# Scores of chunks 5 to 11 of an mLSTM and gated-FFN kernel: fp32 matmuls replaced by stacked fp32r ones

## What is computed

```python
for t in range(S):                      # mLSTM, per batch and head; 2 x 8 heads, S = 768, D = 40
    m_new = np.maximum(f + m, i)
    f_stab, i_stab = np.exp(f + m - m_new), np.exp(i - m_new)
    C = f_stab * C + i_stab * outer(vt, kt);  n = f_stab * n + i_stab * kt
    y[t] = sigmoid(o) * (C @ qt) / max(abs(n @ qt), 1)
x = y as 1536 tokens x 320
x = (1 / (1 + np.exp(-(x @ w_gate))) * (x @ w_val)) @ w_out      # 320 -> 1536 -> 320
return ((x @ w_a) * (x @ w_b)) @ w_out2                          # the same, without a sigmoid
```

## Time and profile before

| | us |
|---|---|
| median of 3 runs (485.88 to 488.06) | 486.16 |
| the profiled execution | 485.53 |
| its span in the trace | 483.7 |
| PE busy | 470.9 (97%) |
| ACT busy | 182.9 (38%) |
| DVE busy | 175.7 (36%) |
| POOL busy | 110.7 (23%) |

### The profile page before, as it was taken

How to read it: one execution, slowest core, us unless ns; L and a number is a source line. 1 busy time by engine, 2 the same in 40 slices (tenths; PEclk the granted TensorE clock), 3 DMA queues, 4 the chain that set the end, 5 groups by cost and what they waited for, 6 DMA issues and landing times.

```text
span 483.7 us, 6541 instructions
## 1 busy us (share of the span) xinstructions
PE 470.9 (97%) x2531; PEld 412.4 (85%) x2531; DVE 175.7 (36%) x339; ACT 182.9 (38%) x345; POOL 110.7 (23%) x97
## 2 busy tenths in 40 slices
PE   7968899999999999999999999999999999999997
PEld 4867789888898988988888888888888888888886
DVE  6754534343454433334322234222222222222223
ACT  4544574643527263423434444222232222222222
POOL 3348855561230302000344443000000000000000
PEclk9996999999999999999999999999999999999999
DMA  5675837423141326000123310000010000100001
GB/s 136 210 216 158 241 125 247 124 68 102 47 132 55 99 74 210 1 0 1 47 93 108 123 47 1 0 1 0 1 55 1 0 1 0 56 1 1 0 1 54
DMA packets 20890, 34.34 MB, mean 71 GB/s; under 512 B 2372, under 2 KB 15068, under 8 KB 20860
## 3 DMA queue, kind: packets, MB, share of 16 engines
q1 hardware_dynamic: 20231, 32.93, 21.8%
q10 hardware_dynamic: 629, 1.00, 0.6%
HBM read 31.85 MB, written 2.04 MB: 70 GB/s over the span
## 4 chain that ended last, share of the span: by engine, by line
PE 89%; DMA 5%; POOL 2%; SPq 2%; issue 1%; DVE 0%; POOLq 0%; DVEq 0%
PE bank L518 53%; PE bank L535 26%; PE bank L446 3%; PE bank L421 3%; DMA levels<-a_scratch 1%; DMA vk<-vk_in 1%; DMA i_row<-i_in 1%; PE bank L437 1%; DMA d_scratch<-d_row 1%; PE bank L500 1%; PE bank L486 1%; DMA bmask<-bm_in 1%; PE bank L459 1%; PE bank L470 1%; POOL w_lo L1008 1%
## 5 line engine op out<-in xcount | busy, mean ns | idle before, releaser
L848 DVE TENSOR_TENSOR h_ff<-bank,s_ff 128x512 f32<-128x512 f32 x72 | 49.8, 691 | 194.3 <-PE bank L518 185.8
L518 PE MATMUL bank<-xt,w_hi 128*128 128x512 f32 x360 | 118.5, 394 | 1.4 <-issue 1.4
L679 ACT CAST h_hi<-h_ff 128x512 fp32r<-128x512 f32 x72 | 44.6, 619 | 133.0 <-DVE h_ff L848 129.9
L672 ACT ACTIVATE s_ff<-bank 128x512 f32<-128x512 f32 x72 | 43.1, 599 | 133.5 <-PE bank L518 133.3
L518 PE MATMUL bank<-xt,w_lo 128*128 128x512 f32 x216 | 84.7, 392 | 0.0
L518 PEld LDWEIGHTS bank<-xt,w_hi 128*128 128x128 f32 x360 | 65.6, 188 | 13.3 <-issue 1.8
L854 DVE TENSOR_TENSOR h_lo<-h_ff,h_hi 128x512 fp32r<-128x512 f32 x72 | 52.1, 724 | 55.4 <-ACT h_hi L679 55.4
L518 PE MATMUL bank<-xt,w_hi_mid 128*128 128x512 f32 x180 | 59.2, 394 | 0.0
L518 PE MATMUL bank<-xt,w_hi_end 128*128 128x512 f32 x180 | 59.2, 394 | 0.0
L518 PEld LDWEIGHTS bank<-xt,w_lo 128*128 128x128 f32 x216 | 40.5, 188 | 8.7
L535 PE MATMUL bank<-w_hi,h_hi 128*128 128x320 f32 x144 | 45.2, 314 | 0.0
(11 more groups left out here) (106 smaller groups left out, 660.7 us busy)
## 6 DMA issues: line engine op xcount, KB each, us to landing
w_raw<-w_in SPq DMA_DIRECT2D x24, 544.0 KB, 4.2
vk<-vk_in SPq DMA_DIRECT2D x12, 344.0 KB, 3.2
levels<-a_scratch SPq DMA_DIRECT2D x8, 512.0 KB
k<-kq_in SPq DMA_DIRECT2D x11, 180.0 KB
y<-rows_t SPq DMA_DIRECT2D x12, 160.0 KB, 1.9
q<-kq_in SPq DMA_DIRECT2D x10, 180.0 KB
q_blk<-q_in SPq DMA_DIRECT2D x22, 60.0 KB
osig_b<-o_in SPq DMA_DIRECT2D x8, 160.0 KB, 3.2
```

The costliest lines, as they stand in the source:

```text
L518: mm = pe.matmul(up_bank(u, gv)[:, :], w_part(low, f, (gv * 3 + kt) * P, P), xt[:, xb * TOK + g * TG:xb * TOK + (g + 1) * TG], start=(j == ...
L672: act.activation(s_ff[u % 2][:, :], up_bank(u, 0)[:, :], ACT.Sigmoid if u < UNITS // 2 else ACT.Copy).then_inc(act_s, 1)
L679: act.copy(h_hi[u % 2][:, :], h_ff[u % 2][:, :]).then_inc(act_h, 1)
L848: dve.tensor_tensor(h_ff[u % 2][:, :], up_bank(u, 1)[:, :], s_ff[u % 2][:, :], ALU.mult).then_inc(dve_h, 1)
```

## The change

Chunks 5 to 11 get another form of the scores. Queries and keys of a chunk are loaded in plain form into `part_raw`, ACT rounds them to fp32r (`part_high`), POOL takes the rest (`part_low`), and SP stores both parts to DRAM (`store_part`). From there SP reads them back stacked along the contraction (`load_stack`): per head 120 partitions hold for the keys high, high, low, and for the queries high, low, high. One fp32r matmul per head, contraction 120, 128 columns, then gives high x high + high x low + low x high. Per chunk this is two loads, two stores and six stacked loads in place of four loads.

`q_stk` and `k_stk` lie where the `q_blk` and `k3` of chunk 4 lay. `part_high` stands on ACT at k = 1 (queries) and k = 2 (keys), behind `h_high`; `part_low` on POOL in the same units, ahead of `w_low`. To make room, `osig_b`, `s_ff` and `h_ff` have one buffer instead of two, with waits to match (the last four lines of the diff are those of `gate(u)` and `hidden(u)`), and `rec` shares `den`.

```diff
+            def load_part(n, q_or_k):
+                rows, width = part_of(q_or_k)
+                wait(sp, pool_part, part_no(n, q_or_k) - 1)
...
+                sp.dma_start(part_raw[0:rows, 0:width], src).then_inc(ld_part, 16)
+            def store_part(n, q_or_k):
+                rows, width = part_of(q_or_k)
+                sp.wait_ge(pool_part, part_no(n, q_or_k))
...
+                sp.dma_start(dst, src.bitcast(F32)).then_inc(st_part, 16)
+            def load_stack(n, q_or_k):
+                sp.wait_ge(pe_s, 2 * n)
+                sp.wait_ge(st_part, 16 * part_no(n, q_or_k))
+                for at in range(3):
...
+                    sp.dma_start(dst.bitcast(F32), src).then_inc(ld_stk, 16)
...
             load_w(4)
-            load_o(5)
+            load_part(ALONE + 1, "q")
             for u in range(3 * (NCH - ALONE) - 2):
                 n, k = piece(u)
-                if k == 0 and n >= ALONE + 2:
+                if k == 0:
                     load_o(n)
+                    store_part(n, "k")
+                    load_stack(n, "k")
+                    if n + 1 < NCH:
+                        load_part(n + 1, "q")
                 if k == 1 and n + 1 < NCH:
                     load_rows(n + 1)
-                    load_q(n + 1)
+                    store_part(n + 1, "q")
+                    load_part(n + 1, "k")
                 if k == 2 and n + 1 < NCH:
                     load_scaled(n + 1)
                     load_v(n + 1)
+                    load_stack(n + 1, "q")
...
+                if n > ALONE:
+                    for h in range(half * HEADS // 2, (half + 1) * HEADS // 2):
+                        at, k_at = (h - half * HEADS // 2) * P, (h % 3 * 3 + h // 3) * P
+                        mm = pe.matmul(st[:, at:at + P], k_stk[:, k_at:k_at + P], q_stk[:, h * P:(h + 1) * P],
+                                       start=True, stop=True)
...
+            def part_high(n, q_or_k):
+                rows, width = part_of(q_or_k)
+                act.wait_ge(ld_part, 16 * part_no(n, q_or_k))
+                wait(act, st_part, 16 * (part_no(n, q_or_k) - 1))
+                act.copy(part[0:rows, 0:width], part_raw[0:rows, 0:width]).then_inc(act_part, 1)
...
+            def part_low(n, q_or_k):
+                pool.wait_ge(act_part, part_no(n, q_or_k))
+                pool.tensor_tensor(part[0:rows, width:2 * width], part_raw[0:rows, 0:width],
+                                   part[0:rows, 0:width].bitcast(F32), ALU.subtract).then_inc(pool_part, 1)
...
-                wait(act, dve_h, u - 1)
+                wait(act, dve_h, u)
-                wait(dve, act_h, u - 1)
+                wait(dve, dve_hlo, u)
```

More of the change, by code:

```diff
@@ L102, in ab @@
                 return stack.enter_context(nc.sbuf_tensor(f"{name}{s}", shape, dt))
+            if s == 0:
+                stacks = ExitStack()
+                stacked.append(stacks.enter_context(nc.sbuf_tensor("q_stk", [TRI, HEADS * P], F32R)))
+                stacked.append(stacks.enter_context(nc.sbuf_tensor("k_stk", [TRI, TRI // HD * 3 * P], F32R)))
+                stacks.close()
+            q_tile, k_tile = ab("q_blk", [TRI, HEADS * P]), ab("k3_", [TRI, 3 * P])
+            if s == 0:
+                ab("k_rest", [TRI, 6 * P])
             rows = ExitStack()
@@ L135, in build @@
         set0 = chunk_set(ctx, 0)
-        levels, arow, q_blk, k3, q3, i_rep, vk, pt, x_raw, x_n, den, rec = zip(set0, set1)
+        levels, arow, q_blk, k3, q3, i_rep, vk, pt, x_raw, x_n, den = zip(set0, set1)
+        q_stk, k_stk = stacked
+        part_raw, part = sb("part_raw", [P, 3 * P]), sb("part", [P, 6 * P], F32R)
         w_hi, w_lo = sb("w_hi", [P, 6 * WC], F32R), sb("w_lo", [P, 6 * WC], F32R)
@@ L139, in build @@
         w_raw = [sb(f"w_raw{i}", [P, WC]) for i in range(RING)]
-        consts = sb("consts", [P, 2 * P])
-        ident = consts[:, 0:P]
-        osig_b = [sb(f"osig_b{i}", [P, DM]) for i in range(2)]
+        ident = sb("ident", [P, P])
+        osig_b = sb("osig_b", [P, DM])
         d_row, m_prev = sb("d_row", [ROWS, CHUNKS]), sb("m_prev", [ROWS, CHUNKS])
@@ L152, in build @@
         h_lo = [sb(f"h_lo{i}", [P, TG], F32R) for i in range(2)]
-        s_ff = [sb(f"s_ff{i}", [P, TG]) for i in range(2)]
-        h_ff = [sb(f"h_ff{i}", [P, TG]) for i in range(2)]
+        s_ff, h_ff = sb("s_ff", [P, TG]), sb("h_ff", [P, TG])
         bank = [ctx.enter_context(nc.psum_tensor(f"bank{i}", [P, 512], F32)) for i in range(8)]
@@ L678, in h_high @@
                 wait(act, pe_d, u - 1)
[L679 removed]
+                act.copy(h_hi[u % 2][:, :], h_ff[:, :]).then_inc(act_h, 1)
             def rows_out(group):
@@ L699, in _ @@
             act.wait_ge(dve_warm, 1)
-            act.activation(s_ff[0][0:1, 0:1], h_hi[0][0:1, 0:1].bitcast(F32), ACT.Sigmoid).then_inc(act_table, 1)
+            act.activation(s_ff[0:1, 0:1], h_hi[0][0:1, 0:1].bitcast(F32), ACT.Sigmoid).then_inc(act_table, 1)
             act.wait_ge(dve_zero, 2)
@@ L747, in _ @@
                 h_high(u)
+                if k in (1, 2) and n + 1 < NCH:
+                    part_high(n + 1, " qk"[k])
                 if k == 0:
@@ L816, in combine @@
                 dve.wait_ge(dve_den, 2 * n + 2)
-                dve.reciprocal(rec[s][:, :], den[s][:, :]).then_inc(dve_rec, 1)
+                dve.reciprocal(den[s][:, :], den[s][:, :]).then_inc(dve_rec, 1)
                 dve.wait_ge(dve_rec, n + 1)
@@ L820, in combine @@
                 dve.tensor_tensor(heads(x_raw[s][:, :], HD), u3[:, :, 0:HD],
-                                  rec[s][:, :].unsqueeze(2).to_broadcast([P, HEADS, HD]),
+                                  den[s][:, :].unsqueeze(2).to_broadcast([P, HEADS, HD]),
                                   ALU.mult).then_inc(dve_y, 1)
@@ L974, in open_x @@
                 s = set_of(n)
-                gate, at = (osig_a, n * DM) if n < ALONE else (osig_b[n % 2], 0)
+                gate, at = (osig_a, n * DM) if n < ALONE else (osig_b, 0)
                 pool.wait_ge(act_o, 1 if n < ALONE else n - 2)
@@ L1066, in _ @@
                         mask(n + 1)
+                if k in (1, 2) and n + 1 < NCH:
+                    part_low(n + 1, " qk"[k])
                 for f in W_AT.get(u, ()):
```

50 lines of the change are left out of this document (38 added, 12 removed).

## The result

The changed kernel took 522.38 us (median of 4 runs, 518.36 to 523.3) against 486.8 for the kernel before: a ratio of 1.0718, 95% interval 1.0673 to 1.0762. The forecast was 487.0, its range 481.5 to 493.5. It was wrong in size and in kind: no rival reached beyond 497. The profiled execution took 523.3 us, its span is 521.5. Executions that ran over 1.5% longer than the fastest of their kernel (one each in runs 4, 5 and 8) are left out of all ratios.

What follows compares the result with a forecast made beforehand. PE almost alone was taken to bound the kernel from 58 us on. A saving of 6.0 us against waits of 1.1, 1.2, 2.5, 1.4 and 1.1 gave +1.3 us, forecast as 487.0 us, range 481.5 to 493.5.

Steps and rivals of the forecast that it cites:

- The saving: Scores of chunks 5 to 11: fp32r matmuls at 0.109 us, 0.87 a chunk instead of 1.73, 6.0 us saved.
- rival 1: Scores' matmuls faster, 0.064 us each: 8.5 us saved, 484.5 us in all; chance 0.15.
- rival 2: Scores' narrow fp32r matmuls run at the fp32 rate: nothing saved, only the waits, 493 us; chance 0.15.
- (a): PE waits for open_x(4), delayed on POOL behind chunk 5's query split: 1.1 us (bounds 0.4 and 1.6).
- (b): Weight load w(6) issued late behind the queries' store, so gate(2) holds up PE: 1.2 us (bounds 0 and 2.5).
- (c): Chunk 5's scores wait for the keys' stack, loaded behind w(6): 2.5 us (bounds 0 and 4).
- (d): Chunk 6's scores wait for the keys' stack: 1.4 us (bounds 0 and 3.4).
- (e): Chunks 7 to 11: round trip of 9.0 against 8.6 to 8.9 us given, waits of 1.1 (bounds 0 and 12).
- stacks 4.0: Time for a chunk's three key stack loads, 552 KB, within the round trip before its scores: 4.0 us.
- rival 3: Keys' store takes 5.0 us rather than 3.0, so five chunks wait 2 more each: 497 us; chance 0.08.
- The rest: Other edits, such as single buffers for s_ff, h_ff and osig_b and rec in den, were to cost nothing.
- the bound of 10: Sign across the kernel: the forecast is wrong if the waits sum to less than 5 or more than 10 us.

Runs made afterwards that it cites:

- run 4: Changed kernel with the new form in chunks 6 to 11 only, splits one unit earlier, stack loads at k = 2, weight loads ahead of stores: 487.39 us.
- run 5: Run 4 with the new form from chunk 7 on, loads of weights 12 on held, tiles aligned: 482.31 us; with chunk 6 also in the new form: 484.24.
- run 8: Kernel before with key and query loads of chunks 5 to 11 issued late: 505.3 us, again 511.26; with loads released later still: 533.58.
- run 1: Changed kernel's buffers, tile places and waits, with the loads and fp32 scores of the kernel before: 488.18 us, ratio 1.0046.
- run 6: d_row allocated ahead of w_hi, which moves tile starts by 32 bytes: 488.04 us in the kernel before, 520.65 in the changed kernel.
- run 2: Changed kernel with parts made for chunk 5 only; chunks 6 to 11 load chunk 5's stacks early: 491.48 us, ratio 1.0121.
- Run 3: Changed kernel with 7 to 17 extra matmuls of 512 columns ahead of each stack wait: 514.26 us, ratio 1.0581.
- run 7: Changed kernel with loads of stale keys, in differently split groups, measured by themselves after chunk 11's scores: 525.04 us, once.

## Why the prediction was wrong, step by step

- **What bounds the kernel: right.** PE alone; every late datum was lost whole.
- **The saving: right.** 0.106 us a matmul, 0.88 a chunk; rivals 1 and 2 fall with it.
- **(a) open_x(4), 1.1:** PE waited 3.2 for it, 1.8 above before. But the wait scatters: kernels with before's order there waited 1.4 to 2.7 (2.1 in the mean of eight traces: before, runs 1, 4, 5, 6 and 8), those with the changed order 2.5 to 3.2 (3.0 in five: after, runs 2, 3, 6 and 7). So some 0.8 is the change's, and the step was about right.
- **(b) w(6), 1.2:** right in mechanism, and 1.5 measured. Its cast began at 70.39 with ACT idle 6.58 before it, not near 67, but PE came as much later. A second weight block was late in the same way (PE waited 2.0 for its gate until 101.48), which no term had.
- **(c) and (d), keys of chunks 5 and 6, 2.5 and 1.4:** measured 4.0 and 4.2. The store landed in 7.7 and 6.0 us, priced as bytes in a backlog at some 2.0 each, and the stack load took 6.4 and 6.6 where I had 4.0 (for 552 KB; three loads of 180 are 540, which changes 0.1 us).
- **(e) chunks 7 to 11, 1.1 in sum:** measured 3.5 + 1.8 + 1.6 + 1.5 + 1.8 = 10.2. The term that failed is "stacks 4.0". The stacks took 6.4, 5.2, 5.3, 5.2 and 5.6, together 7.7 over, most of the 9.1 that the term was short. The store was right (2.9 in four of five; 3.5 in chunk 7). The 4.0 came from a line through two landings, a store's of 160 KB and a load's of 344 KB; alone a load of 180 KB takes 2.7 to 3.1 here. A round trip of 9.0 against a lead of 8.6 to 8.9 is decided by its error; I should have put far more on rival 3. That rival had the size of the waits (10) but the wrong leg and a chance of 0.08.
- **The step that is missing: what a wait costs beyond itself.** I wrote that a new wait of PE is "lost whole" and stopped there. Behind the waits the granted clock fell to 1.2 GHz: up to 20 us, over half of the loss. Before's own clock row shows it, low in the fourth slice, behind its wait of 3.6 us for `vk`. The Trainium skill (TensorE: Matmul & The Clock Gate, The HAM clock gate) says that an idle PE falls to half clock; the trace agrees (3.26 us for eight `up` matmuls of 1.84). Run 3 shows it from one side, with work put into the waits, and run 8 from the other, with waits put into the kernel before. I had looked at that page for the price of a matmul alone.
- **The rest:** single s_ff, h_ff and osig_b cost nothing (run 1), as said. No step had the shift of the tiles, 1.6 us in the kernel before.

The waits' sum of 25 us (24 above before's) broke the bound of 10 that I had named. Open: why one wait of 2 us lowers the clock and another does not.

## What to carry to other kernels

A PE-bound kernel can pay for a wait twice, in its length and in the clock behind it; a gain of 0.9 us a chunk is not worth a datum that is late by 1. Before adding a round trip through DRAM, add up its legs from rows of the same kind (loads from loads, with the transfers that are issued behind them), and start it a whole unit earlier than the sum asks: the same exchange cost 36 us with a lead that my sum found 0.1 to 0.4 us short, and won 4 us (five chunks) with a unit more and the weight loads out of its way. Leave out the chunks whose lead other loads take.

## What the runs showed of the hardware that I had not expected

- Waits of 1.3 to 4 us can be enough to lower the clock (1.3 in run 7's trace), though one of 3.1 did not in run 6: the changed kernel spent some 40 us more at 1.2 GHz (twice the 20 us withheld).
- An fp32r matmul of 128 columns with new stationary columns each time: 0.106 us.
- A matmul of 512 columns takes 395 ns in place of 390 where its moving tile starts at an odd multiple of 32 bytes and its stationary one at a multiple of 64; both odd or both even give 390.
- 540 KB from DRAM land in 4.8 to 4.9 us, as one load or three, and in 6.2 behind a weight load of 544 KB. A queries' stack behind its keys' stack (1020 KB) landed 7.8 us after its last issue in run 5 (chunk 11) and 9.6 in run 4, with three weight loads behind it.
